# The token steps of the dense expert units written out on TensorE, with fixed token columns in place of a register-addressed loop

## The reference

```python
def _moe_ref(x, w_gate, w1, w2):             # x: 3072 x 384, 8 experts, F = 1024
    P = np.exp(logits)
    for _ in range(8):
        P /= P.sum(1, keepdims=True) + 1e-09
        P /= P.sum(0, keepdims=True) + 1e-09
        P *= N / E
    for e in range(E):
        h = np.maximum(x @ w1[e], 0.0)
        ye = h @ w2[e]
        out += P[:, e:e + 1] * ye

def _moe2_ref(...):                          # the second one, top 2 of 8
    for e in range(E):
        for k in range(2):
            h = np.maximum(x[mask] @ w1[e], 0.0)
            out[mask] += top2_w[mask, k, None] * (h @ w2[e])
```

## Time and profile before

| | us |
|---|---|
| median of 3 runs (2534.53 to 2537.75) | 2536.76 |
| the profiled execution | 2525.23 |
| its span | 2523.5 |
| TensorE busy in the span (96%) | 2426.4 |
| VectorE busy | 1042.4 |
| ScalarE busy | 648.6 |
| GpSimd busy | 502.8 |

### The profile page before, as it was taken

How to read it: one execution, slowest core, us unless ns; L and a number is a source line. 1 busy time by engine, 2 the same in 40 slices (tenths; PEclk the granted TensorE clock), 3 DMA queues, 4 the chain that set the end, 5 groups by cost and what they waited for, 6 DMA issues and landing times.

```text
span 2523.5 us, 40444 instructions
## 1 busy us (share of the span) xinstructions
PE 2426.4 (96%) x14404; PEld 2412.0 (96%) x14404; DVE 1042.4 (41%) x2039; ACT 648.6 (26%) x1165; POOL 502.8 (20%) x327
## 2 busy tenths in 40 slices
PE   6989999999999999999999999999957999999997
PEld 6989999999999999999999999999957999999997
DVE  8992354333333333333333333333553444444443
ACT  3441111111111111111111111112433444444442
POOL 2112101011010110110101101101343333333332
PEclk9999999999999999999999999999978999999999
DMA  5452000000000000000000000001314556555653
GB/s 137 111 149 86 0 25 25 0 25 0 25 25 0 25 25 0 25 0 25 25 0 25 25 0 25 0 25 44 38 19 138 173 153 190 147 172 165 168 173 53
DMA packets 45907, 155.54 MB, mean 62 GB/s; under 512 B 12992, under 2 KB 32320, under 8 KB 37936
## 3 DMA queue, kind: packets, MB, share of 16 engines
q1 hardware_dynamic: 29984, 127.89, 16.1%
q0 software_dynamic: 15888, 27.19, 6.1%
HBM read 130.23 MB, written 24.82 MB: 61 GB/s over the span
## 4 chain that ended last, share of the span: by engine, by line
PE 90%; DVE 6%; issue 2%; DMA 1%; ACT 1%; POOL 0%; DVEq 0%; ACTq 0%; SPq 0%; POOLq 0%
PE bank L1085 43%; PE bank L1076 43%; DVE inv L651 1%; DVE decay L645 1%; PE bank L1190 1%; DVE probs L659 1%; PE bank L994 1%; PE bank L1132 0%; DMA slots<-record,places 0%; DVE state L683 0%; PE bank L1126 0%; DVE stsum L682 0%; ACT xrow L528 0%; DVE x_lo L665 0%; DVE acc L786 0%
## 5 line engine op out<-in xcount | busy, mean ns | idle before, releaser
L1085 PE MATMUL bank<-w_hi,h_hi 128*128 128x384 f32 x2088 | 709.9, 340 | 4.1 <-DVE h_lo L747 4.1
L1085 PE MATMUL bank<-w_hi,h_lo 128*128 128x384 f32 x2088 | 700.1, 335 | 0.0
L1085 PE MATMUL bank<-w_lo,h_hi 128*128 128x384 f32 x2088 | 700.1, 335 | 0.0
L516 ACT ACTIVATE h_hi<-bank 128x384 fp32r<-128x384 f32 x512 | 251.6, 491 | 1338.2 <-PE bank L1076 1337.0
L1076 PE MATMUL bank<-x_hi,w_hi 128*128 (+1 forms) x1536 | 522.1, 340 | 0.0
L1076 PE MATMUL bank<-x_lo,w_hi 128*128 (+1 forms) x1536 | 520.5, 339 | 0.0
L1076 PE MATMUL bank<-x_hi,w_lo 128*128 (+1 forms) x1536 | 520.4, 339 | 0.0
L747 DVE SCALAR_TENSOR_TENSOR h_lo<-bank,h_hi 128x384 fp32r<-128x384 f32 x512 | 284.2, 557 | 391.4 <-ACT h_hi L516 374.9
L758 DVE SCALAR_TENSOR_TENSOR acc<-bank,route,acc 128x384 f32 (+1 forms) x336 | 186.7, 611 | 589.8 <-PE bank L1085 589.8
L1085 PEld LDWEIGHTS bank<-w_hi,h_hi 128*128 128x128 f32 x2088 | 392.5, 188 | 4.6 <-issue 4.6
L1085 PEld LDWEIGHTS bank<-w_lo,h_hi 128*128 128x128 f32 x2088 | 393.0, 188 | 0.0
(11 more groups left out here) (154 smaller groups left out, 1909.4 us busy)
## 6 DMA issues: line engine op xcount, KB each, us to landing
raw<-wts SPq DMA_DIRECT2D x62, 1536.0 KB, 6.4
qka_sb<-qka SPq DMA_DIRECT2D x48, 288.0 KB, 4.8
out_dram<-zrow SPq DMA_DIRECT2D x1, 5376.0 KB, 18.0
v_sb<-v SPq DMA_DIRECT2D x24, 192.0 KB, 2.5
x<-acc SPq DMA_DIRECT2D x8, 576.0 KB
xg<-x,slot_in POOLq DMA_INDIRECT x69, 5.1
out_dram<-ys,slot_out POOLq DMA_INDIRECT x69, 4.6
x<-zrow SPq DMA_DIRECT2D x1, 768.0 KB, 18.7
```

The lines of the kernel that those rows point to most:

```text
L516: act.activation(h_hi[:, f], ps_h[f][:, 0:TW], ACT.Relu).then_inc(s_hh, 1)
L1085: mm = pe.matmul(ps_o[s][:, 0:DM], hx, w, start=(first and n == 0), stop=(last and n == 2))
```

## The change

`dense_unit` runs its eight token steps in a Python loop, so the steps stand in the program one after the other and `tok` is a constant slice. `routed_step` gets constant columns in all eight steps. The loop over `e` stays, so `u` is still a register in it: the values of the waits are still computed. Nothing changes on the other engines, and the order of the matmuls and the semaphores of each are the same.

```diff
@@ dense_unit
-                with pe.Fori(0, TS) as j:
+                for j in range(TS):
                     g = u * TS + j
-                    tok = bass.ts(j, TW)
+                    tok = slice(j * TW, (j + 1) * TW)
                     pe.wait_ge(s_spl, 2 * u + 1 + PRIMED)
                     for f in range(FC):
                         up(f, *w1, lambda k: x_hi[:, k, tok], lambda k: x_lo[:, k, tok]).then_inc(s_hd, 1)
@@ routed_step
-                tok = bass.ds(j * TW, TW)
+                tok = slice(j * TW, (j + 1) * TW)
@@
-            for j in range(3):
-                routed_step(j)
-            with pe.Fori(3, TS) as j:
+            for j in range(TS):
                 routed_step(j)
```

## The result

The changed kernel takes 2539.17 us in the median of 20 runs (2536.18 to 2546.12), the kernel before 2536.51 us in 20 runs taken with them (2531.25 to 2542.12). The ratio is 1.0013 with a 95% interval of 1.0007 to 1.0019: by the ratio 3.3 us slower. That can be told from no difference at all, but it lies within the 0.2% that the prediction called no change. Forecast were +3.3 us and 2540.0.

A forecast was written before the change was run, and what follows sets the result against it. TensorE, busy for 96% of the span, was taken to bound the kernel. Matmuls 0, branches and registers 0, straight code 0 and five jumps 3.3 us gave 2536.76 + 3.3 = 2540.0 us, range 2533 to 2549.

The forecast's parts named there:

- Matmuls at no change: In the `up` matmuls of the 125 changed steps, constant columns save nothing: 125 x 0.00 us.
- the 0.10 us: Rival: register addresses cost each `up` 0.10 us a step, so the change is 12.5 us faster, 2524.3; chance 0.08.
- Registers and branches of the token loop at no gain: Removed register work and token-loop branches in TensorE's sequencer gain 0, being covered by 16 queued matmuls of `down`.
- Straight code at no cost: Fetching the new written-out matmuls, a packet every 15 to 20 us, costs 0 in straight code.
- The jump misses: At five jumps back of the loop over `e`, the 1,152-matmul body's start is no longer held and must be fetched.
- M: Price of one instruction fetch at a jump back of the loop over `e`, taken as 3.5 us.
- late by 0.65 us: At each of five jumps the first `up` comes 3.5 - 2.85 = 0.65 us late, +3.3 us in all.
- The cover of 2.85 us: Time at each jump during which queued matmuls keep the array busy: 2.75 + 0.2, less 0.1 for the wait.
- Packets: Instruction queue q8 would carry some 90 to 110 packets instead of 21, 45 of them for the longer program.
- rival 2: Dear jumps: fetch 4.4 us or more, or a second piece, 2544.5 (chance 0.28); with clock falling, 2561 (0.05).
- The second piece that has to be fetched: At each jump, another fetch soon after the first could stop the array 1.5 us or longer; within the 0.28 chance.
- the fall of the clock: Behind long stops at jumps, slower `down` adds 1.8 us each; with 3 us stops 24 us, 2561; chance 0.05.

The follow-up runs named there:

- the kernel without the loop: The changed kernel with the loop over `e` written out too, so no jump back is left in the dense stage; ratio to before 0.9996 (0.9987 to 1.0005).
- the bodies of 1,526 and 1,826 instructions: Four and five steps of each dense unit written out, the rest looped, against before; single runs 2526.2 us to 2529.8 and 2559.7 us to 2528.8.

## Why the prediction was right, step by step

- **Matmuls at no change.** Right. The control inside the trace of before, where constant and register columns stand side by side, decided it against the 0.10 us that the earlier trace rows seemed to offer. In the loop over `e` and in unit 14 of the changed kernel `up` is 6.36 us, but for the five behind a jump (6.46 by the starts).
- **Registers and branches of the token loop at no gain.** Right: 105 taken branches and all register work for the columns are gone, and the stretch without jumps is 1300.5 us in either form.
- **Straight code at no cost.** Right, and shown at its hardest by the kernel without the loop.
- **The jump misses.** Right: 3.3 to 3.8 us for each in both profiles. From the earlier trace rows alone it could be suspected, not known; the limit now lies between the bodies of 1,526 and 1,826 instructions.
- **M = 3.5 us, late by 0.65 us, +3.3 us.** Measured were 3.32 to 3.82 us in the first profile, and 0.73 us late on average there (0.55 in the second): 3.7 and 2.7 us in all, against 3.3 by the timed ratio. The cover of 2.85 us was right within 0.1: 3.82 - 1.04 = 2.78 and 3.32 - 0.49 = 2.83 us. Not in the sum were the 0.1 us a jump of the slow second matmul; with them the stretch grew by 4.1 and 3.1 us. The closeness of M is luck in part, because it was picked between 2.8 and 4.4, from DMAs of other queues, and each 0.1 us of it counts 0.5 us. The packet's own 1.2 us was a fair price (0.9 to 1.4 measured); the rest of M, 1.0 to 1.2 us ahead of the packet and 1.3 to 1.5 behind it, no row of before could show.
- **Packets.** 90 to 110 were forecast, 99 came. The 45 of it for the longer program agree with its 11,422 instructions in blocks of 256; by the 165 bytes for a matmul that the prediction goes by it would have been 50.
- **The rivals.** M itself never came to the 4.4 us of rival 2; the longest branch of any kernel was 3.9. The second piece that has to be fetched and the fall of the clock are real, but in other kernels: they need a loop that starts close before the end of a block. In the changed kernel it starts 217 instructions before one. I had the mechanism as a chance of 0.28 plus 0.05 and gave no condition that a reader could have looked up in the program; the place of the start is that condition.

## What to carry to other kernels

Register addresses, loop branches and waits on computed values cost TensorE nothing in these kernels, where its sequencer stands ahead by more than they take (2.75 us against some 0.7); look for a step in the same trace that is already written the other way before costing them. Writing a loop out inside another loop can push the outer body past what the engine holds, here between 1,526 and 1,826 instructions (7 and 9 blocks), and then each jump back costs 3.3 to 3.8 us less the cover of the queue. If such a loop must stay, its start should not lie just ahead of a block's end; otherwise write all of it out, which cost nothing here.

## What the runs showed of the hardware that I had not expected

- The same loop, moved by 564 instructions, made the kernel go from 1.0013 to 1.0081 of before. At a jump the next block is fetched only after the one before it has come: with the boundary 13 instructions behind the jump's target the second stop was 2.25 to 2.52 us, and with the boundary between the first weight load and its matmul 2.8 to 3.3 us.
- The stop doesn't show as a wait for a DMA. It is in the length of the branch's own record (a median of 3.44 us instead of 0.208) and in idle time put down to issue.
- Unit 15 takes 127.0 to 136.2 us in 14 profiles, whichever way it is written. Two profiles of before differ by 4.7 us in it, more than the whole change. A stretch that holds the change and repeats to 0.02 us in before tells more than either span.
